# Chained attention, routed experts and dense layer: the TensorE expert loop and its exit rearranged, with one read and some subtractions moved

## The chip, the cores and the metric

The kernel runs on one core of one Trainium2 chip. The metric is the device time of one execution in microseconds (us). Before the change it is 740.41 us, the median of 3 runs (739.77 to 741.19).

## The reference, cut to what matters

Three layers follow each other. The first is a linear attention with decay (4 batches, 8 heads, 768 steps, head width 48), which gives 3072 rows of 384 numbers. The second is a routed layer of 8 experts, the third a dense layer:

```python
# second layer: x is (3072, 384); w1 (8, 384, 1024); w2 (8, 1024, 384)
do_compute = (x @ w_skip) > 0
e_idx = argmax(xc @ w_gate)                  # xc: the rows with do_compute
h = maximum(xc[mask] @ w1[e], 0)             # for each expert e
y[mask] = gate_w[mask] * (h @ w2[e])
out[do_compute] = xc + y
# third layer: w_in (384, 2048), w_out (2048, 384)
h = x @ w_in
g = h * clip(h + 3, 0, 6) / 6
result = g @ w_out
```

## The kernel before, in words

Every engine has a program of its own; they meet at semaphores only. All large products are made of three fp32r products of high and low parts: `three` (L866 to L869) issues high times high (L867), high times low (L868) and low times high (L869). A high part is made by ScalarE (a copy that rounds), a low part by VectorE (raw minus high).

**Stage 1** (about 0 to 170 us) is the attention and the routing. It writes the rows x to the scratch tensor `x_scratch` and counts how many tiles of 256 rows the experts need. With these inputs the plan has 8 tiles, one for each expert: the hidden products L867 into `bank_A` stand in the profile 144 times, which is 18 for each tile.

**Stage 2** (about 170 to 316 us) is the expert loop. Each engine runs `expert_loop` (L290): two tiles written out (j = 0 and 1), a loop over j = 2 to 7 by pairs, and behind a test `n_tiles > 8` a second loop for tiles 8 to 19, which is jumped over here. In the TensorE program one tile (`experts`, L880) has three parts: the hidden products for 8 pieces f, `rows_T` (L871), which transposes the gathered rows of the next tile, and the products with w2 for the two halves t = 0 (`bank_L`) and t = 1 (`bank_P`). That is 126 products in a tile. SyncE (`experts`, L368) reads the weights of tile j: w1 into `raw1` in three transfers (L378) once VectorE has made all low parts of w1 of tile j - 1, and w2 into `raw2` in one (L380) once the low parts of w2 of tile j - 1 are there. POOL gathers the rows of tile j + 1 (L505, two indirect transfers) and scatters the results of tile j (L537). VectorE evicts the results of a half with `yg` (L1222), ScalarE turns `raw1` into w1_hi (L659).

Behind the loop SyncE reads w_in into `wi_raw` (L388, eight transfers), waits for POOL's `s_before_last` (the scatters of the tile before the last have landed), reads the first 512 rows of x into `m_first` (L391, four transfers), and then reads w_out into `wo_raw` (L394, eight transfers of 384 KB).

**The passage to stage 3** is what the change is about. The rows of the last tile are not read back from `x_scratch`. TensorE transposes `m_first` (L961, 4 x 3 products, into the banks `bank_rT`, `bank_YT`, `bank_X`) and adds the last tile's results to them: `gain_hi` and `gain_lo` of the halves t = 0, 1, multiplied with the 0/1 matrix `goes_to` (L968, 12 products of 512 columns). Its order is t outside, then high and low, then the three banks kc, and each bank's `s_mT` is given at its last product. ScalarE makes `gain_hi` (L714) once both halves have been evicted (L1222), VectorE `gain_lo` (L1256). Then ScalarE makes `mT_hi` for each kc (L682) and VectorE `mT_lo` (L1230), and the first dense block may begin. ScalarE has before that made w_in's high parts 0 to 11 (`win_hi`, L646). VectorE makes w_in's low part 0 (`win_lo`, L1179) ahead of the three `mT_lo` and part 1 behind them.

**Stage 3** (about 331 to 745 us) is the dense layer in 6 blocks of 512 rows, each over 16 pieces f: 9 products of 512 columns for piece f of the hidden layer (it waits for `s_wilo` in the first block), then 12 products of 384 columns with w_out for piece f - 2 (`second`, L917). In the first block VectorE also makes w_out's low part f (L1184) and w_in's low part f + 2, and ScalarE w_out's high part f (L650) and w_in's high part f + 12. ScalarE waits for the whole of w_out (`s_wo`, L698) before the first of these.

Of the kernel before, what the change touches and what calls it, by code (L numbers as in the profile page):

```python
# [12 lines left out]
P = 128  # L13
B, H, S, HD = 4, 8, 768, 48
D = H * HD
# [5 lines left out]
KC = D // P  # L21
E, F1 = 8, 1024
G1 = F1 // P
F2 = 2048
G2 = F2 // P
TT = 256
TH = TT // P
MAXT = (N + E * (TT - 1)) // TT
# [6 lines left out]
BT = BLK // P  # L35
# [7 lines left out]
C_W1, C_W2 = (1, 2, 3), (1, 2, 3, 4)  # L43
W2_PARTS = len(C_W2)
W_PARTS = 8
HI_FIRST, LO_FIRST = 12, 2
SETS = 3
LATE = 3
GW = 32
# [14 lines left out]
def wait(eng, sem, value):  # L64

    if isinstance(value, int) and value <= 0:
        return
    eng.wait_ge(sem, value)


def chained_moe_program(nc, r, k, v, w, u, w_skip, w_gate, w1, w2, w_in, w_out, out, x_dram, slot_dram):
    ctx = ExitStack()
    with ctx:
# [90 lines left out]
        m_first = nc.alloc_sbuf_tensor_at("m_first", [P, BT, D], F32, offset=at_hi)  # L164
# [3 lines left out]
        goes_to, gain_hi, gain_lo = [], [], []  # L168
# [7 lines left out]
        wo_raw = nc.alloc_sbuf_tensor_at("wo_raw", [P, G2, D], F32, offset=at_lo)  # L176
# [6 lines left out]
        class Region:  # L183
# [60 lines left out]
        g = [de(f"g{i}", [P, BLK]) for i in range(2)]  # L244
# [45 lines left out]
        def expert_loop(eng, n_tiles, step):  # L290

            for i in range(2):
                step(i, 0, i)
            with eng.Fori(1, E // 2) as m:
                for i in range(2):
                    step(m * 2 + i, m, i)
            with eng.If(n_tiles > E):
                with eng.Fori(E // 2, MAXT // 2) as m:
                    for i in range(2):
                        step(m * 2 + i, m, i)  # L300
# [15 lines left out]
        def _(eng):  # L316
# [23 lines left out]
            for c in range(NC):  # L340
                for b in range(B):
                    n = c * B + b
# [22 lines left out]
            eng.dma_start(who_all[:, :, :], slots_by_p).then_inc(s_who_all, 16)  # L365
            n_tiles = tiles_planned(eng)

            def experts(j, m, i):  # L368
                if isinstance(j, int) and j == 0:
                    return  # L370
                with eng.If(n_tiles > j):
                    e = eng.value_load(plan[0:1, bass.ds(j, 1)], min_val=0, max_val=E - 1)
                    wait(eng, s_w1lo, KC * j)
                    if isinstance(j, int) and j == 1:
                        for done in s_xg[0]:
                            eng.wait_ge(done, 16)
                    for kc in range(KC):
                        eng.dma_start(raw1[:, kc, :], w1[bass.ds(e, 1), kc * P:(kc + 1) * P, :].rearrange("a p f -> p (a f)")).then_inc(s_raw1[kc], 16)  # L378
                    wait(eng, s_w2lo, G1 * j)
                    eng.dma_start(raw2[:, :, :], w2[bass.ds(e, 1), :, :].rearrange("a (g p) n -> p (a g) n", p=P)).then_inc(s_raw2, 16)  # L380

            expert_loop(eng, n_tiles, experts)

            wi_dram = w_in.rearrange("(k p) f -> p k f", p=P)
            wo_dram = w_out.rearrange("(g p) n -> p g n", p=P)
            for part in range(W_PARTS):
                own_f = slice(part * F2 // W_PARTS, (part + 1) * F2 // W_PARTS)
                eng.dma_start(wi_raw[:, :, own_f], wi_dram[:, :, own_f]).then_inc(s_wi, 16)  # L388
            eng.wait_ge(s_before_last, 1)
            for t in range(BT):  # L390
                eng.dma_start(m_first[:, t, :], x_dram[t * P:(t + 1) * P, :]).then_inc(s_m0[t], 16)  # L391
            for part in range(W_PARTS):
                own_g = slice(part * G2 // W_PARTS, (part + 1) * G2 // W_PARTS)
                eng.dma_start(wo_raw[:, own_g, :], wo_dram[:, own_g, :]).then_inc(s_wo, 16)  # L394
            eng.wait_ge(s_moe, 1)

            def load_m(blk):
# [323 lines left out]
        def _(eng):  # L721
# [144 lines left out]
            def three(dst, a_hi, a_lo, b_hi, b_lo, start, stop):  # L866
                eng.matmul(dst, a_hi, b_hi, start=start, stop=False)  # L867
                eng.matmul(dst, a_hi, b_lo, start=False, stop=False)  # L868
                return eng.matmul(dst, a_lo, b_hi, start=False, stop=stop)  # L869

            def rows_T(j, m, i):  # L871

                wait(eng, s_gTlo, TH * j)
                for t in range(TH):
                    eng.wait_ge(s_xg[i][t], 16 * (m + 1))
                    for kc in range(KC):
                        a = eng.transpose(p_xgT[t][:, kc * P:(kc + 1) * P], xg[i][:, t, kc * P:(kc + 1) * P], ident[:, :])
                    a.then_inc(s_gT, 1)

            def experts(j, m, i):  # L880
                with eng.If(n_tiles > j):
                    eng.wait_ge(s_w1lo, KC * (j + 1))
                    eng.wait_ge(s_gTlo, TH * (j + 1))
                    for f in range(G1):

                        wait(eng, s_hlo, G1 * j + (f - 1 if f < 2 else f - 2))
                        for kc in range(KC):
                            piece = slice(f * P, (f + 1) * P)
                            a = three(p_h[f % 3][:, 0:TT], w1_hi[:, kc, piece], w1_lo[:, kc, piece],
                                      xgT_hi[:, kc, :], xgT_lo[:, kc, :], kc == 0, kc == KC - 1)  # L890
                        a.then_inc(s_h, 1)
                    with eng.If(n_tiles > j + 1):
                        rows_T(j + 1, m + i, 1 - i)
                    for t in range(TH):
                        wait(eng, s_y2ev, TH * j + t + 1 - TH)
                        for f in range(G1):
                            if t == 0:
                                eng.wait_ge(s_hlo, G1 * j + f + 1)
                                eng.wait_ge(s_w2lo, G1 * j + f + 1)
                            tok = slice(t * P, (t + 1) * P)  # L900
                            a = three(p_y[t][:, 0:D], hT_hi[:, f, tok], hT_lo[:, f, tok], w2_hi[:, f, :], w2_lo[:, f, :],
                                      f == 0, f == G1 - 1)
                        if t < TH - 1:
                            a.then_inc(s_y2t, 1)
                    a.then_inc(s_y2, 1)

            rows_T(0, 0, 0)
            n_tiles = tiles_planned(eng)
            expert_loop(eng, n_tiles, experts)

            def rows_mT(kc, done):
                eng.wait_ge(s_mlo, done)
# [42 lines left out]


            eng.sem_inc(s_O, SHIFT)
            for t in range(BT):
                eng.wait_ge(s_m0[t], 16)
                for kc in range(KC):  # L960
                    eng.matmul(p_first_mT[kc][:, t * P:(t + 1) * P], m_first[:, t, kc * P:(kc + 1) * P], ident[:, :], start=t == 0, stop=False,  # L961
                               is_transpose=True, skip_group_check=True)
            for t in range(TH):
                for gain, done in ((gain_hi, s_gain_hi), (gain_lo, s_gain_lo)):
                    eng.wait_ge(done, t + 1)
                    final = gain is gain_lo and t == TH - 1
                    for kc in range(KC):
                        a = eng.matmul(p_first_mT[kc], gain[t][:, kc * P:(kc + 1) * P], goes_to[t][:, :], start=False, stop=final,  # L968
                                       skip_group_check=True)
                        if final:  # L970
                            a.then_inc(s_mT, 1)
            dense_loop(eng, blocks)


# [1 line left out]
        def _(eng):  # L976
# [198 lines left out]
            def win_lo(f):  # L1175

                piece = slice(f * P, (f + 1) * P)
                eng.wait_ge(s_wihi, f + 1)
                eng.tensor_tensor(wi_lo[:, :, piece], wi_raw[:, :, piece], wi_hi[:, :, piece].bitcast(F32), ALU.subtract).then_inc(s_wilo, 1)  # L1179
# [74 lines left out]
            for t in range(TH):  # L1254
                eng.wait_ge(s_gain_hi, t + 1)
                eng.scalar_tensor_tensor(gain_lo[t][:, :], p_y[t][:, 0:D], last_w[:, t:t + 1], gain_hi[t][:, :].bitcast(F32),  # L1256
                                         ALU.mult, ALU.subtract).then_inc(s_gain_lo, 1)
            win_lo(0)
            for kc in range(KC):
                rows_lo(0, kc, kc, p_first_mT[kc])  # L1260
            for f in range(1, LO_FIRST):
                win_lo(f)
            dense_loop(eng, blocks)

# [22 lines left out]
```

## Time and profile before

| | |
|---|---|
| median of 3 runs | 740.41 us |
| the profiled execution | 747.21 us |
| its span, first to last instruction | 745.4 us |
| TensorE busy with products | 699.1 us (94%) |
| VectorE / ScalarE / POOL busy | 385.0 / 323.6 / 140.5 us |
| mean granted clock of TensorE | 0.981 of full speed |
| moved by DMA | 65.61 MB, 88 GB/s on average |

The profiled execution is 1.8 us longer than its span and 6.8 us longer than the median of the runs without the profiler. PE is TensorE with its products, PEld its weight loads, DVE is VectorE, ACT ScalarE, SPq the queue of SyncE, POOLq that of POOL. Times in the trace are counted from the first instruction. "Idle before" is what an engine sat idle ahead of an instruction, with what ended it. "issue" stands where it waited for nothing that the profile shows.

### The profile page before, as it was taken

The numbers are of one execution on the slowest core, as the hardware profiler recorded it, in microseconds if no ns is written. First come the engines' busy times: TensorE is split into PE (matmuls) and PEld (weight loads), VectorE is DVE, ScalarE is ACT, GpSimd is POOL, SyncE is SP. The second block draws the span as 40 slices with busy tenths as digits, with TensorE's granted clock in tenths as the row PEclk, the third lists the DMA queues.
The fourth block names the chain that finished last, engine by engine and source line by source line (L and its number), as shares of the span: only waits on it lengthen the run. The fifth ranks groups of instructions, "written<-read, shape, count | busy, mean of one in ns | idle before, by whom it ended". The sixth has DMA issues, their size and how long they took to land.

```text
span 745.4 us, 13560 instructions
## 1 busy us (share of the span) xinstructions
PE 699.1 (94%) x5103; PEld 637.9 (86%) x5103; DVE 385.0 (52%) x767; ACT 323.6 (43%) x703; POOL 140.5 (19%) x189
## 2 busy tenths in 40 slices
PE   5999999938999999959999999999999999999997
PEld 3888888827999999948999899899998999998996
DVE  5576667565888888526554333333243333333332
ACT  3766666624555555625443233333232333323222
POOL 8647866441222222100000000000000000000000
PEclk9999999977999999989999999999999999999999
DMA  9888887113666666930002000200010020001001
GB/s 156 150 182 168 180 159 151 44 36 113 207 213 224 214 218 217 320 128 2 0 1 85 1 0 1 85 1 0 24 63 1 0 85 1 1 0 43 1 1 42
DMA packets 106988, 65.61 MB, mean 88 GB/s; under 512 B 79938, under 2 KB 102756, under 8 KB 106928
## 3 DMA queue, kind: packets, MB, share of 16 engines
q1 hardware_dynamic: 102864, 60.18, 30.4%
q0 software_dynamic: 2816, 4.60, 2.0%
q8 instruction: 39, 0.64, 0.4%
q10 hardware_dynamic: 1248, 0.02, 0.1%
q14 instruction: 21, 0.17, 0.1%
HBM read 53.69 MB, written 12.80 MB: 89 GB/s over the span
## 4 chain that ended last, share of the span: by engine, by line
PE 84%; ACT 4%; issue 4%; DVE 3%; DMA 2%; another core or an unknown queue 1%; POOL 1%; POOLq 0%; DVEq 0%; ACTq 0%; SPq 0%
PE bank_A L868 8%; PE bank_A L869 8%; PE bank_A L867 8%; PE bank_A L805 4%; PE bank_L L867 4%; PE bank_L L869 4%; PE bank_L L868 4%; PE bank_P L869 4%; PE bank_P L868 4%; PE bank_P L867 4%; PE bank_kT L868 3%; PE bank_kT L869 3%; PE bank_kT L867 3%; ACT bank_A L588 3%; PE bank_YT L869 3%
## 5 line engine op out<-in xcount | busy, mean ns | idle before, releaser
L1239 DVE TENSOR_TENSOR g_lo<-g,g_hi 128x512 fp32r<-128x512 f32 x96 | 66.5, 692 | 67.1 <-ACT g_hi L693 67.1
L693 ACT ACTIVATE g_hi<-g 128x512 fp32r<-128x512 f32 x96 | 60.7, 632 | 72.7 <-DVE g L1237 72.7
L1237 DVE SCALAR_TENSOR_TENSOR g<-cut,bank_A 128x512 f32<-128x512 f32 x60 | 41.2, 687 | 92.1 <-ACT cut L690 92.1
L690 ACT ACTIVATE cut<-bank_A 128x512 f32<-128x512 f32 x60 | 35.8, 597 | 102.3 <-PE bank_A L869 101.8
L867 PE MATMUL bank_A<-mT_hi,wi_hi 128*128 128x512 f32 x180 | 70.1, 389 | 1.8 <-DVE wi_lo L1179 1.8
L869 PE MATMUL bank_A<-mT_hi,wi_lo 128*128 128x512 f32 x180 | 71.0, 395 | 0.0
L868 PE MATMUL bank_A<-mT_lo,wi_hi 128*128 128x512 f32 x180 | 70.9, 394 | 0.0
L588 ACT ACTIVATE bank_A<-ident,own 128x128 f32<-128x128 f32 x192 | 59.2, 358 | 6.2 <-DVE A_sb L1030 3.2
L1237 DVE SCALAR_TENSOR_TENSOR g<-cut,bank_kT 128x512 f32<-128x512 f32 x36 | 24.8, 688 | 68.0 <-ACT cut L690 68.0
L690 ACT ACTIVATE cut<-bank_kT 128x512 f32<-128x512 f32 x36 | 21.5, 597 | 71.6 <-PE bank_kT L869 71.6
L1030 DVE TENSOR_TENSOR A_sb<-bank_A,upto 128x512 f32<-128x512 f32 x48 | 30.9, 685 | 23.7 <-PE bank_A L805 18.3
L867 PE MATMUL bank_kT<-mT_hi,wi_hi 128*128 128x512 f32 x108 | 42.1, 390 | 1.0 <-DVE mT_lo L1230 1.0
L867 PE MATMUL bank_A<-xgT_hi,w_hi 128*128 128x256 f32 x144 | 41.6, 289 | 1.3 <-DVE xgT_lo L1196 1.3
L869 PE MATMUL bank_kT<-mT_hi,wi_lo 128*128 128x512 f32 x108 | 42.7, 396 | 0.0
L868 PE MATMUL bank_kT<-mT_lo,wi_hi 128*128 128x512 f32 x108 | 42.6, 395 | 0.0
L672 ACT ACTIVATE hT_hi<-bank_A 128x256 fp32r<-128x256 f32 x48 | 18.4, 383 | 55.2 <-PE bank_A L869 54.2
L869 PE MATMUL bank_A<-xgT_hi,w_lo 128*128 128x256 f32 x144 | 41.5, 288 | 0.0
L868 PE MATMUL bank_A<-xgT_lo,w_hi 128*128 128x256 f32 x144 | 41.5, 288 | 0.0
L867 PEld LDWEIGHTS bank_A<-mT_hi,wi_hi 128*128 128x128 f32 x180 | 33.8, 188 | 7.9 <-issue 2.2
L869 PEld LDWEIGHTS bank_A<-mT_hi,wi_lo 128*128 128x128 f32 x180 | 33.7, 187 | 7.2
L868 PEld LDWEIGHTS bank_A<-mT_lo,wi_hi 128*128 128x128 f32 x180 | 33.8, 188 | 6.0
L805 PE MATMUL bank_A<-rT,kT 64*128 64x128 f32 x384 | 28.8, 290 | 8.3 <-ACT bank_A L588 5.7
(240 smaller groups left out, 1853.1 us busy)
## 6 DMA issues: line engine op xcount, KB each, us to landing
raw<-in_moe_w_dram SPq DMA_DIRECT2D x24, 512.0 KB
raw<-in_moe_w_dram SPq DMA_DIRECT2D x7, 1536.0 KB
r_in<-in_r_dram SPq DMA_DIRECT2D x24, 192.0 KB, 4.5
k_in<-in_k_dram SPq DMA_DIRECT2D x24, 192.0 KB, 4.5
v_in<-in_v_dram SPq DMA_DIRECT2D x24, 192.0 KB, 3.6
x_scratch<-y_sb SPq DMA_DIRECT2D x24, 192.0 KB, 2.5
out_dram<-o_sb SPq DMA_DIRECT2D x12, 384.0 KB, 2.8
m_in<-x_scratch SPq DMA_DIRECT2D x5, 768.0 KB, 5.4
```

The source lines that it names most:

```text
L588: a = eng.activation(p_A[:, o, q * P:(q + 1) * P], ident[:, :], ACT.Copy, scale=own[n % 2][:, 2 * q + o:2 * q + o + 1])
L672: eng.activation(hT_hi[:, f, :], p_h[f % 3][:, 0:TT], ACT.Relu).then_inc(s_hhi, 1)
L690: eng.activation(cut[f % 2][:, :], p_H[f % 3][:, :], ACT.Relu, bias=0.5, scale=1.0 / 6.0).then_inc(s_cut, 1)
L693: eng.activation(g_hi[f % 4][:, :], g[f % 2][:, :], ACT.Copy).then_inc(s_ghi, 1)
L805: m = eng.matmul(p_A[:, o, q * P:(q + 1) * P], kT[i][half, q, :], rT[i][half, q, :], start=False, stop=True, skip_group_check=True)
L867: eng.matmul(dst, a_hi, b_hi, start=start, stop=False)
L868: eng.matmul(dst, a_hi, b_lo, start=False, stop=False)
L869: return eng.matmul(dst, a_lo, b_hi, start=False, stop=stop)
L1030: eng.tensor_tensor(A_sb[i][:, o, :, :], p_A[:, o, :].rearrange("s (q t) -> s q t", q=NPAIR), mask, ALU.mult).then_inc(s_Aev, 1)
L1237: eng.scalar_tensor_tensor(g[f % 2][:, :], cut[f % 2][:, :], 1.0, p_H[f % 3][:, :], ALU.min, ALU.mult).then_inc(s_g, 1)
L1239: eng.tensor_tensor(g_lo[f % 4][:, :], g[f % 2][:, :], g_hi[f % 4][:, :].bitcast(F32), ALU.subtract).then_inc(s_glo, 1)
```

## The change: what it does

It does five things. (1) TensorE no longer uses `expert_loop`: tile 0 and tile 1 are written out, and one loop over pairs follows for m = 1 to 9, with the tests `n_tiles > 2m` and `n_tiles > 2m + 1` inside it, so with 8 tiles the passes m = 4 to 9 find nothing to do. The other engines keep `expert_loop`. (2) The transposes of `m_first` stand inside the tile, behind its last product, under the test `n_tiles < j + 2`. (3) The gain products run kc outside: all four of `bank_rT`, `s_mT`, then the next bank. (4) SyncE reads w_out behind the weights of tile 1 rather than behind `m_first`. (5) VectorE makes four low parts of w_in ahead of `mT_lo`, two behind, and in the first block the part f + 6.

```diff
-HI_FIRST, LO_FIRST = 12, 2
+HI_FIRST, LO_EARLY, LO_FIRST = 12, 4, 6
...
@@ SyncE, experts(j, m, i)
                     wait(eng, s_w2lo, G1 * j)
                     eng.dma_start(raw2[:, :, :], ...).then_inc(s_raw2, 16)
+                if isinstance(j, int):
+                    for part in range(W_PARTS):
+                        own_g = slice(part * G2 // W_PARTS, (part + 1) * G2 // W_PARTS)
+                        eng.dma_start(wo_raw[:, own_g, :], wo_dram[:, own_g, :]).then_inc(s_wo, 16)
...
             for t in range(BT):
                 eng.dma_start(m_first[:, t, :], x_dram[t * P:(t + 1) * P, :]).then_inc(s_m0[t], 16)
-            for part in range(W_PARTS):
-                own_g = slice(part * G2 // W_PARTS, (part + 1) * G2 // W_PARTS)
-                eng.dma_start(wo_raw[:, own_g, :], wo_dram[:, own_g, :]).then_inc(s_wo, 16)
...
@@ TensorE
+            def first_rows_T():
+                for t in range(BT):
+                    eng.wait_ge(s_m0[t], 16)
+                    for kc in range(KC):
+                        eng.matmul(p_first_mT[kc][:, t * P:(t + 1) * P], m_first[:, t, kc * P:(kc + 1) * P], ident[:, :], start=t == 0, stop=False,
+                                   is_transpose=True, skip_group_check=True)
...
             def experts(j, m, i):
-                with eng.If(n_tiles > j):
...
                     a.then_inc(s_y2, 1)
+                with eng.If(n_tiles < j + 2):
+                    first_rows_T()
...
-            expert_loop(eng, n_tiles, experts)
+            experts(0, 0, 0)
+            with eng.If(n_tiles > 1):
+                experts(1, 0, 1)
+            with eng.Fori(1, MAXT // 2) as m:
+                with eng.If(n_tiles > m * 2):
+                    experts(m * 2, m, 0)
+                    with eng.If(n_tiles > m * 2 + 1):
+                        experts(m * 2 + 1, m, 1)
...
             eng.sem_inc(s_O, SHIFT)
-            for t in range(BT):
-                eng.wait_ge(s_m0[t], 16)
-                ...
-            for t in range(TH):
-                for gain, done in ((gain_hi, s_gain_hi), (gain_lo, s_gain_lo)):
-                    eng.wait_ge(done, t + 1)
-                    final = gain is gain_lo and t == TH - 1
-                    for kc in range(KC):
-                        ...
+            for kc in range(KC):
+                for t in range(TH):
+                    for gain, done in ((gain_hi, s_gain_hi), (gain_lo, s_gain_lo)):
+                        eng.wait_ge(done, t + 1)
+                        a = eng.matmul(p_first_mT[kc], gain[t][:, kc * P:(kc + 1) * P], goes_to[t][:, :], start=False,
+                                       stop=gain is gain_lo and t == TH - 1, skip_group_check=True)
+                a.then_inc(s_mT, 1)
...
@@ VectorE
-            win_lo(0)
+            for f in range(LO_EARLY):
+                win_lo(f)
             for kc in range(KC):
                 rows_lo(0, kc, kc, p_first_mT[kc])
-            for f in range(1, LO_FIRST):
+            for f in range(LO_EARLY, LO_FIRST):
                 win_lo(f)
```

## Rows read from the trace of the kernel before

**Rows 1.** The page: span and busy time of each engine.

```profile
span 745.4 us, 13560 instructions
PE 699.1 (94%) x5103; PEld 637.9 (86%) x5103; DVE 385.0 (52%) x767; ACT 323.6 (43%) x703; POOL 140.5 (19%) x189
```

**Rows 2.** Windows: length, busy time of each engine, clock, DMA share, GB/s.

```profile
400.00:745.00 345.00, 340.52 (x1735) 308.65 (x1734) 123.37 (x184) 109.45 (x184) 0.00 (x0) 1.00 0.07 23
316.40:330.80 14.40, 6.18 (x26) 4.96 (x25) 3.07 (x6) 2.53 (x5) 0.97 (x1) 0.76 0.52 177
190.00:194.00 4.00, 4.00 (x27) 4.00 (x27) 2.52 (x7) 0.00 (x0) 1.04 (x1) 1.00 1.03 350
```

**Rows 3.** Waits of TensorE: waited for, us in total, times, longest.

```profile
PE bank_X L961 <- issue: 3.7, 1, 3.7
PE bank_rT L961 <- issue: 3.5, 1, 3.5
PE bank_A L867 <- DVE wi_lo L1179: 1.8, 1, 1.8
PE bank_kT L877 <- DMA xg<-x_scratch,who: 1.2, 1, 1.2
```

**Rows 4.** Timeline of TensorE at the passage: start, duration, instruction, idle before.

```profile
316.07 0.34 PE L869 MATMUL bank_P<-w_hi,hT_lo 128*128 128x384 f32 x1
319.86 0.30 PE L961 MATMUL bank_rT<-ident,m_first 128*128 128x128 f32 x1 [3.45 <-issue]
...
324.32 0.37 PE L961 MATMUL bank_X<-ident,m_first 128*128 128x128 f32 x1 [3.72 <-issue]
...
329.36 0.39 PE L968 MATMUL bank_X<-goes_to,gain_lo 128*128 128x512 f32 x1
...
332.71 0.40 PE L869 MATMUL bank_kT<-mT_hi,wi_lo 128*128 128x512 f32 x1
```

**Rows 5.** Timelines of VectorE and ScalarE at the passage.

```profile
316.45 0.62 DVE L1222 SCALAR_TENSOR_TENSOR yg<-bank_P,who,xg 128x384 f32<-128x384 f32 x1 [3.47 <-PE bank_P L869]
318.25 0.61 DVE L1256 SCALAR_TENSOR_TENSOR gain_lo<-bank_P,last_w,gain_hi 128x384 fp32r<-128x384 f32 x1
318.77 0.55 DVE L1179 TENSOR_TENSOR wi_lo<-wi_raw,wi_hi 128x384 fp32r<-128x384 f32 x1
329.95 0.69 DVE L1230 TENSOR_TENSOR mT_lo<-bank_rT,mT_hi 128x512 fp32r<-128x512 f32 x1 [10.63 <-ACT mT_hi L682]
...
329.32 0.60 ACT L682 ACTIVATE mT_hi<-bank_rT 128x512 fp32r<-128x512 f32 x1 [11.17 <-PE bank_rT L968]
```

**Rows 6.** DMA queue q8 (packets, MB, share): span, then 175 to 246, 317 to 326 us.

```profile
q8 instruction: 39, 0.64, 0.4%
...
q8 instruction: 4, 0.07, 0.4%
...
q8 instruction: 2, 0.03, 1.5%
```

**Rows 7.** Timelines of SyncE's queue and of ScalarE around tiles 1 and 2.

```profile
185.55 0.39 SPq L380 DMA_DIRECT2D raw<-in_moe_w_dram  x1
189.58 1.37 SPq L378 DMA_DIRECT2D raw<-in_moe_w_dram  x3
...
202.46 2.94 ACT L659 ACTIVATE w_hi<-raw 128x1024 fp32r<-128x1024 f32 x3
```

**Rows 8.** POOL's second gather for tile 2, its reader, DMA landings 193:211, 175:246, 299:317.

```profile
198.10 1.00 POOL L505 DMA_INDIRECT xg<-x_scratch,who  x1 [0.31 <-issue]
...
201.89 0.49 PE L877 MATMUL bank_kT<-ident,xg 128*128 128x128 f32 x3
...
xg<-x_scratch,who POOLq DMA_INDIRECT x2, 2.9
...
x_scratch<-yg,whom POOLq DMA_INDIRECT x7, 4.0
...
x_scratch<-yg,whom POOLq DMA_INDIRECT x3, 6.3
```

More of the change, by code:

```diff
@@ L366, in _ @@
             n_tiles = tiles_planned(eng)
+            wo_dram = w_out.rearrange("(g p) n -> p g n", p=P)
             def experts(j, m, i):
@@ L380, in experts @@
                     eng.dma_start(raw2[:, :, :], w2[bass.ds(e, 1), :, :].rearrange("a (g p) n -> p (a g) n", p=P)).then_inc(s_raw2, 16)
+                if isinstance(j, int):
+                    for part in range(W_PARTS):
+                        own_g = slice(part * G2 // W_PARTS, (part + 1) * G2 // W_PARTS)
+                        eng.dma_start(wo_raw[:, own_g, :], wo_dram[:, own_g, :]).then_inc(s_wo, 16)
             expert_loop(eng, n_tiles, experts)
             wi_dram = w_in.rearrange("(k p) f -> p k f", p=P)
-            wo_dram = w_out.rearrange("(g p) n -> p g n", p=P)
             for part in range(W_PARTS):
@@ L878, in rows_T @@
                     a.then_inc(s_gT, 1)
-            def experts(j, m, i):
-                with eng.If(n_tiles > j):
-                    eng.wait_ge(s_w1lo, KC * (j + 1))
-                    eng.wait_ge(s_gTlo, TH * (j + 1))
-                    for f in range(G1):
-                        wait(eng, s_hlo, G1 * j + (f - 1 if f < 2 else f - 2))
-                        for kc in range(KC):
[L888 to L893, printed above, removed]
-                    for t in range(TH):
[L895 to L905, printed above, removed]
@@ new lines, in first_rows_T @@
+            def first_rows_T():
[4 more added lines that the diff above has]
+                                   is_transpose=True, skip_group_check=True)
+            def experts(j, m, i):
+                eng.wait_ge(s_w1lo, KC * (j + 1))
+                eng.wait_ge(s_gTlo, TH * (j + 1))
+                for f in range(G1):
+                    wait(eng, s_hlo, G1 * j + (f - 1 if f < 2 else f - 2))
+                    for kc in range(KC):
+                        piece = slice(f * P, (f + 1) * P)
+                        a = three(p_h[f % 3][:, 0:TT], w1_hi[:, kc, piece], w1_lo[:, kc, piece],
+                                  xgT_hi[:, kc, :], xgT_lo[:, kc, :], kc == 0, kc == KC - 1)
+                    a.then_inc(s_h, 1)
+                with eng.If(n_tiles > j + 1):
+                    rows_T(j + 1, m + i, 1 - i)
+                for t in range(TH):
+                    wait(eng, s_y2ev, TH * j + t + 1 - TH)
+                    for f in range(G1):
+                        if t == 0:
+                            eng.wait_ge(s_hlo, G1 * j + f + 1)
+                            eng.wait_ge(s_w2lo, G1 * j + f + 1)
+                        tok = slice(t * P, (t + 1) * P)
+                        a = three(p_y[t][:, 0:D], hT_hi[:, f, tok], hT_lo[:, f, tok], w2_hi[:, f, :], w2_lo[:, f, :],
+                                  f == 0, f == G1 - 1)
+                    if t < TH - 1:
+                        a.then_inc(s_y2t, 1)
+                a.then_inc(s_y2, 1)
+                with eng.If(n_tiles < j + 2):
+                    first_rows_T()
@@ L957, in _ @@
             eng.sem_inc(s_O, SHIFT)
-            for t in range(BT):
-                eng.wait_ge(s_m0[t], 16)
[L960 to L963, printed above, removed]
-                for gain, done in ((gain_hi, s_gain_hi), (gain_lo, s_gain_lo)):
-                    eng.wait_ge(done, t + 1)
-                    final = gain is gain_lo and t == TH - 1
[L967 to L971, printed above, removed]
+            for kc in range(KC):
+                for t in range(TH):
+                    for gain, done in ((gain_hi, s_gain_hi), (gain_lo, s_gain_lo)):
[3 more added lines that the diff above has]
+                a.then_inc(s_mT, 1)
             dense_loop(eng, blocks)
```

## The prediction

> **What bounds the kernel now.** I read the page first: TensorE is busy with products for 94% of the span, no other engine for more than 52% [rows 1]. So a microsecond is won only where TensorE stands still or runs slowly. The windows show where that is: from 400 us on it misses 4.5 of 345 us at full clock, and in tiles 0 to 7 hardly anything, but between 316.4 and 330.8 us it is busy for 6.2 of 14.4 us, at a mean clock of 0.76 [rows 2]. That is the passage from the last expert tile to the dense layer. The waits say what it stood for there: twice, 3.5 and 3.7 us, for nothing that the profile shows ("issue"), both at the transposes of `m_first`; later 1.8 us for w_in's low part of piece 2 [rows 3].
>
> An engine that waits for nothing may be waiting for its own code. The queue q8 carries 39 packets and 0.64 MB [rows 6], 16 KB each. Products and weight loads together are 2 x 5103 instructions [rows 1], so q8 carries 63 bytes for each: it is TensorE's code, brought in blocks. Four packets came in 175 to 246 us, one for each tile; none in 246 to 317 us, when the loop ran its second and third pass; and two in 317 to 326 us [rows 6], just where the two stalls are. A pass of two tiles is then held while it repeats, and the jump over the unused second loop, about 36 KB of code by the count of its products, lands outside what is held. The first block arrives at 319.86, five transposes run, and the next one is missing until 324.32 [rows 4].
>
> **The change, part by part.** I call the end of the last tile E: its last product starts at 316.07 and ends at 316.41 [rows 4].
>
> (1) and (2), the loop and the transposes. The transposes follow the last product in the same piece of code, so they run at once: five took from 319.86 to 320.60 (324.32 less the stall of 3.72), 0.3 us for one and 0.11 for each further one [rows 4]; 12 end at about 317.9. Then the sequencer makes six empty passes. No row shows the price of one. From below it is nothing seen: TensorE crosses a tile's tests and branches without a gap, since its queue is full. From above I take the 3.7 us of a missing block [rows 3] for each. I take it near the lower end, below 0.5 us, because the blocks of the loop's head and tail are both held when the loop ends, as they were in passes two and three [rows 6]. The cover: the last half tile is 24 products, 4.2 us, which need only been issued, and the gains aren't ready before 317.7. The sequencer should be through the tile's code at about 313, so 4.6 us are there for six passes, or 0.75 us each, at no cost. If that cover is gone, every further 0.1 us a pass costs 0.6 us. The Trainium skill prices a branch (Advanced Engine Details and Errata, Control Flow Timing) at about 51 ns, with a comparison at 108 ns; six passes of two each would by that estimate be 1.9 us, which no run here shows.
>
> The chain to the dense layer, then, is that of the gains. `yg` of the second half runs at 316.45, the last `gain_lo` at 318.25 to 318.86 [rows 5]; the change touches neither. **(3)** With kc outside, three of bank 0's four gain products are done by then, and the last ends at about 319.35 (0.39 us, as at 329.36 [rows 4]). ScalarE's `mT_hi` takes 0.60: 320.0. **(5)** VectorE now makes four low parts first, from 318.77, of 0.47 us each in a row (0.55 alone [rows 5]): 320.65, so `mT_lo` 0 is done at 321.35 rather than 320.65, and 1 and 2 at 0.61 us intervals, 322.0 and 322.6. The other eight gain products end at 321.2, also before the first `mT_lo`: the new order costs nothing, VectorE sets the pace. The nine products of piece 0 start at 321.5 and the last three after `mT_lo` 2: piece 0 ends at 323.6. Before, its last product started at 332.71 and ended at 333.1 [rows 4]. **Saved: 9.5 us.** In it are the two stalls (7.2 us [rows 3]), and the half clock that followed them: with TensorE idle for some 1 us in place of 7, I expect the clock to stay at 2.4 GHz.
>
> In the first block, piece 2 waited 1.8 us for its low part, which stood behind those of block 0's `g` on VectorE [rows 3]. Parts 0 to 5 now exist before, and f + 6 is made in the same slots, so the wait goes. Next in line is w_out's low part 0, needed after piece 2; VectorE reaches it some 1 us before TensorE does. **Saved: 1.8 us.**
>
> (4) w_out. Where it was, it filled the DMA queues during the passage; that is part of why the blocks came late. Where it goes, eight transfers of 384 KB, 3.1 MB, stand in SyncE's program behind the issue at 185.55 and ahead of the wait and the three w1 transfers of tile 2, now issued at 189.58 [rows 7]. At the 350 GB/s of that stretch [rows 2] w_out takes 9 us. The queue then holds w2 of tile 1 (1.6 MB), w_out and w1 of tile 2 (1.6 MB), 18 us with the gathers between them, so tile 2's w1 lands from 203 to 206.3; ScalarE wants it at 202.46 [rows 7]. High part 1.0, low part 1.2 and the gathered rows' low parts 1.0 behind it end at 209.5. TensorE wants them at 210.5, with 1 us to spare. The gather of tile 2 has nothing to spare: issued at 198.10, with 2.9 us to landing it is there at 201.0, and TensorE reads it at 201.89 [rows 8]. In a full queue a scatter lands after 6.3 us instead of 4.0 [rows 8]. The same 2.3 us here make 203.3, 1.4 us late, and TensorE stands for it with the second half of its tile behind. Bounds: nothing (the queue drains in time) and about 5 us (scatter, gather and w1 all late, as in tile 3 to 4, where a late gather cost 1.2 [rows 3]). I take **1.5 us lost**. The 0.6 us of issue time for each of the eight is SyncE's and hides nothing else.
>
> The sum: -9.5 - 1.8 + 1.5 = **-9.8 us**. Against the profiled execution, 747.2, that makes 737.4; its excess of 6.8 us over the median I leave alone, so the median goes from 740.4 to **730.6 us**.
>
> **The rivals.**
> *A. One code stall is left, or w_out costs its upper bound.* The exit of the loop may still need a block that isn't held, or VectorE's code may be late. That costs up to 3.7 us, less what the wait for the gains covers; with 5 us for w_out both give 730.6 + 3.7 + 3.5 = 737.8 at most, and 734 to 735 for either alone. For it: blocks came only one ahead of use (the second stall). Against: the code behind the loop follows it directly. Chance 0.20.
>
> *B. The empty passes fetch code: slower.* The pair is now about 39 KB, as each tile has 12 transposes more. It covers four blocks, and the one behind is fetched too. If only four are held, which is all that the trace proves, then each pass throws out what the next needs. Price: six passes at 3.7 us [rows 3] are 22.3 us, from 313 to 335.4. Then 12 gain products at the half clock and piece 0 end at about 342.7, against 333.1 before: +9.6 - 1.8 + 1.5, about 749.7 us. It decides at 0.75 us a pass, and turns the sum positive at about 2.3 us a pass. Against it: no packet in three passes, the last with a fourth block already brought. The Trainium skill (Runtime: NRT & Kernel Launch, Instruction fetch mechanics) has a rule that speaks for it: a taken branch whose target lies outside a window of two blocks forces a fetch. By this rule each empty pass would fetch at both its jumps, twice the price, 772 us; but the trace disagrees, with a 36 KB loop repeated without a packet. Chance of both forms 0.05.
>
> *C. The stalls are not the code's place but its volume.* If the passage needs two blocks at 3.6 us wherever it stands, only the 1.8 us and the lighter queue are won, and w_out's price is paid: about 739.5 to 741. For it: the second stall came when the DMA was emptying. Against: the transposes now lie in blocks that have run. Chance 0.04.
>
> **How the numbers follow.** The forecast as summed has 0.71, with 728 to 733 as its own range: w_out at nothing, and a clock that saves 1 us more, below; 2 us more for w_out or the passes above. Rival A reaches 737.8. I take 728.0 to 738.0, which leaves out B, C and a tail. A measurement of this kernel tells 0.2%, 1.5 us, from no change. Faster by more: 0.92; within: 0.03 (most of C); slower: 0.05 (B).
>
> **What would show it.** Right: the "issue" waits at the transposes gone, these directly behind the last product of `bank_P`; clock near 1 in the 14 us behind E; first product with `mT_hi` some 5 us behind E (before 14.4); no wait on `wi_lo`; DMA full from 187 to about 205 us, with a wait on `xg` in tile 1 of 1 to 2 us. Wrong: q8 packets inside the expert loop after its first pass, or several at its end (B); an "issue" wait ahead of the gain products (A); TensorE waiting at the start of tile 2 for `w_lo` or `xgT_lo` (w_out dearer than I think).

## The result, and the profile after

The changed kernel takes 737.39 us (median of 5 runs, 736.86 to 737.46) against 741.14 us before (5 runs, 739.77 to 741.64): a ratio of 0.9952, 95% interval [0.9938, 0.9967]. That is 3.7 us faster, where 9.8 us had been forecast. The sign and the range held; the size of the gain did not.

The two profiled executions differ by 9.8 us all the same, 745.4 against 735.6 us of span. That is a trap. The first product of tile 0 (before, then after) shows it:

```profile
173.18 0.55 PE L867 MATMUL bank_A<-xgT_hi,w_hi 128*128 128x256 f32 x1 [1.26 <-DVE xgT_lo L1196]
```

```profile
166.62 0.55 PE L869 MATMUL bank_A<-xgT_hi,w_hi 128*128 128x256 f32 x1 [1.26 <-DVE xgT_lo L1207]
```

6.6 of the 9.8 us lie in stage 1, whose code the change does not touch. Of these, 4.5 us are waits of TensorE for ScalarE's `diagonal` (L588 before, L590 after), first before, then after:

```profile
PE bank_A L805 <- ACT bank_A L588: 5.7, 10, 1.1
```

```profile
PE bank_A L807 <- ACT bank_A L590: 1.2, 3, 0.5
```

Tile 0 starts at 166.6 us in this one trace and at 172.5 to 176.0 in the other thirteen of both kernels and their variants. What sets it was not found. The three later comparisons ran on three chips, and before takes 747 to 748 us in all of them; on which chip the first comparison ran is not recorded. So each experiment is read against the before of its own comparison, and by stretches of the trace.

I cut each trace at three points: the first product of tile 0, the end E of tile 7's last product, and the first product with w_out. What follows that product takes 406.3 to 406.4 us in every trace, before included. The stretches, from the timeline of TensorE (us):

| | tile 0 to E | first gain product | end of piece 0 | first w_out product |
|---|---|---|---|---|
| before, first profile | 143.2 | E + 9.2 | E + 16.7 | E + 22.7 |
| before, second profile | 142.9 | E + 8.5 | E + 16.2 | E + 22.2 |
| changed | 148.1 | E + 3.65 | E + 10.6 | E + 14.5 |
| changed, second profile | 148.2 | E + 3.65 | E + 10.6 | E + 14.5 |

So the expert stage lost 4.9 us, and the passage up to the first w_out product won 8.2. The sum is 3.3 us, near the 3.7 of the medians.

Not all of the 4.9 us is the change's doing. In every trace tile 0 begins at a granted clock of 0.5, which lasts 4.0 to 6.1 us from its first product: 4.7 in the first profile of before, 5.5 in that of the changed kernel. TensorE works at half pace for that long, so for this reason alone the stage can differ by about 1 us between two traces. It takes 142.9 to 143.9 us in the eight traces where w_out is read elsewhere, and 147.4 to 148.2 in the six where it is read behind tile 1. The means are 4.4 us apart. The first 10 us of tile 0, before and then after (columns as in [rows 2]; the granted clock is the third number from the end):

```profile
173.18:183.18 10.00, 10.00 (x66) 10.00 (x67) 5.65 (x12) 4.91 (x13) 0.00 (x0) 0.77 0.39 150
166.62:176.62 10.00, 10.00 (x63) 10.00 (x64) 5.30 (x12) 4.79 (x12) 0.00 (x0) 0.73 0.41 154
```

**The passage after**, TensorE's timeline (the rows that answer to [rows 4]):

```profile
314.41 0.34 PE L871 MATMUL bank_P<-w_hi,hT_lo 128*128 128x384 f32 x1
314.59 0.27 PE L887 MATMUL bank_rT<-ident,m_first 128*128 128x128 f32 x1
...
315.79 0.27 PE L887 MATMUL bank_X<-ident,m_first 128*128 128x128 f32 x1
318.40 0.47 PE L980 MATMUL bank_rT<-goes_to,gain_hi 128*128 128x512 f32 x1 [2.34 <-issue]
...
319.41 0.63 PE L980 MATMUL bank_rT<-goes_to,gain_lo 128*128 128x512 f32 x1
...
324.95 0.39 PE L871 MATMUL bank_kT<-mT_hi,wi_lo 128*128 128x512 f32 x1
...
329.27 0.33 PE L869 MATMUL bank_YT<-wo_hi,g_hi 128*128 128x384 f32 x1
```

The first transpose starts 0.18 us behind the start of the last product, and both stalls of [rows 3] are gone. A new one of 2.34 us stands ahead of the gain products. It is of the kind "issue" again, although the gains were ready: the last `gain_lo` ends at 317.20. Most of the gain products then start 0.43 us apart, not 0.23: the granted clock is 0.5 from 318.85 to 322.3 us. VectorE (the rows that answer to [rows 5]) no longer sets the pace:

```profile
316.59 0.61 DVE L1267 SCALAR_TENSOR_TENSOR gain_lo<-bank_P,last_w,gain_hi 128x384 fp32r<-128x384 f32 x1
317.12 1.95 DVE L1190 TENSOR_TENSOR wi_lo<-wi_raw,wi_hi 128x384 fp32r<-128x384 f32 x4
320.71 0.69 DVE L1241 TENSOR_TENSOR mT_lo<-bank_rT,mT_hi 128x512 fp32r<-128x512 f32 x1 [1.64 <-ACT mT_hi L684]
```

**The expert stage after.** The gather of tile 2 comes late. TensorE's timeline, the landings of 179 to 205 us, and two windows (columns as in [rows 2]) show it:

```profile
197.79 0.52 PE L879 MATMUL bank_rT<-ident,xg 128*128 128x128 f32 x3 [2.29 <-DMA xg<-x_scratch,who]
```

```profile
xg<-x_scratch,who POOLq DMA_INDIRECT x2, 6.8
```

```profile
197.00:199.00 2.00, 0.89 (x7) 0.69 (x7) 0.00 (x0) 0.15 (x1) 0.00 (x0) 1.00 1.04 398
199.00:203.00 4.00, 4.00 (x16) 4.00 (x15) 3.06 (x3) 3.74 (x5) 0.00 (x0) 0.57 1.03 371
```

The gather takes 6.8 us to landing instead of 2.9 [rows 8]. TensorE stands for 2.3 us, and for another 0.3 at the second half. Behind this the granted clock is 0.57 on the mean of 4 us, in a part of the tile where it had been 1: 3.4 us at half clock, in which 1.7 us are lost. Together that is 4.3 of the 4.4 us. The transposes of successive tiles start 20.06 and 19.74 us apart here, 17.6 in a tile that nothing disturbs.

Code: q8 has 37 packets in the changed kernel for 39 before.

### The profile page after: what moved, and what is told of

It is laid out like the page before. It is cut to its first block, busy times and chain, and to the rows that moved or that the text cites. A ratio compares the mean times of both kernels' runs of the same rounds, so it can differ in the third digit from the quotient of the medians.

```text
span 735.6 us, 13594 instructions
## 1 busy us (share of the span) xinstructions
PE 700.2 (95%) x5103; PEld 639.5 (87%) x5103; DVE 383.7 (52%) x767; ACT 324.3 (44%) x703; POOL 141.0 (19%) x189
## 4 chain that ended last, share of the span: by engine, by line
PE 90%; DVE 2%; DMA 2%; ACT 2%; issue 2%; POOL 1%; POOLq 0%; DVEq 0%; SPq 0%; ACTq 0%
PE bank_A L870 8%; PE bank_A L871 8%; PE bank_A L869 8%; PE bank_A L807 4%; PE bank_L L869 4%; PE bank_L L871 4%; PE bank_L L870 4%; PE bank_P L871 4%; PE bank_P L870 4%; PE bank_P L869 4%; PE bank_kT L870 3%; PE bank_kT L871 3%; PE bank_kT L869 3%; PE bank_YT L871 3%; PE bank_YT L870 3%; PE bank_YT L869 3%
## 5 line engine op out<-in xcount | busy, mean ns | idle before, releaser
L590 ACT ACTIVATE bank_A<-ident,own 128x128 f32<-128x128 f32 x192 | 59.1, 359 | 5.5 <-DVE A_sb L1041 3.0
L1218 DVE TENSOR_TENSOR w_lo<-raw,w_hi 128x384 fp32r<-128x384 f32 x64 | 35.9, 561 | 0.0
```

Of the source, the lines that this page charges most:

```text
L590: a = eng.activation(p_A[:, o, q * P:(q + 1) * P], ident[:, :], ACT.Copy, scale=own[n % 2][:, 2 * q + o:2 * q + o + 1])
L1218: eng.tensor_tensor(w2_lo[:, f, :], raw2[:, f, :], w2_hi[:, f, :].bitcast(F32), ALU.subtract).then_inc(s_w2lo, 1)
```

## The experiments

**1. The kernel before, again** (no edit).

> The kernel before, unchanged, for a second profile. Theory T: its profiled execution of before was 6.6 us long in stage 1 by chance (first hidden product of tile 0 at 173.18 us against 166.62 us in the changed kernel, the waits of L805 for ScalarE 5.7 us against 1.2), and the change itself is worth 3 to 4 us. Then the time is the same as before within 0.2%, the span about 739, tile 0 starts at about 166.6, and both issue stalls at the transposes are there, 7 us together. Rival R: the issue stalls were long by chance in that one execution. Then tile 0 starts near 173 here too and the stalls come to less than 4 us.

Measured: 747.71 us against 747.14 (1.0007 [0.9995, 1.0018]); tile 0 starts at 174.82, the issue stalls are 3.55 and 2.90 us. The stalls are no accident of one execution, as T had it. But stage 1 is as long here as in the first profile, in this kernel and in the others of the comparison (173.3 to 173.9): that part of T missed. It is the profile of the changed kernel that has the short stage 1. The timed runs of before in the first comparison (739.8 to 741.6 us) lie 6 us under its profiled execution of 747.2, so they probably have it short too; no trace shows it, and why was not tried.

**2. w_out back at its old place**, in the changed kernel.

```diff
@@ SyncE, experts(j, m, i)
-                if isinstance(j, int):
-                    for part in range(W_PARTS):
-                        own_g = slice(part * G2 // W_PARTS, (part + 1) * G2 // W_PARTS)
-                        eng.dma_start(wo_raw[:, own_g, :], wo_dram[:, own_g, :]).then_inc(s_wo, 16)
@@ SyncE, behind the reads of m_first
+            for part in range(W_PARTS):
+                own_g = slice(part * G2 // W_PARTS, (part + 1) * G2 // W_PARTS)
+                eng.dma_start(wo_raw[:, own_g, :], wo_dram[:, own_g, :]).then_inc(s_wo, 16)
```

> The changed kernel with part 4 undone: w_out is read behind m_first again. Theory T: w_out behind tile 1 costs 4.9 us of the expert stage (from tile 0's first product to the end of tile 7 143.2 us before, 148.1 after), and the passage no longer needs a quiet DMA since its code is held. Then this takes about 732.5 us, 8 to 9 below before, with no wait of the transposes and no wait on xg in tile 1 over 0.5 us. Rival R: it was the w_out traffic at the passage that made the passage slow, so with it there again the issue wait before the gain products grows from 2.3 to 4 us or more and the time is 736 us or more.

Measured: 738.74 us against 747.14, 0.9887 [0.9871, 0.9904], 8.4 us below before. Tile 0 to E is 143.7 us, and the stall ahead of the gain products is 2.34 us to the hundredth. With the code in place, w_out's traffic costs the passage nothing: piece 0 ends at E + 9.0 here and also where w_out is out of the way (experiment 4). The time is over R's 736 us, but only because before is longer here too (see 4); R's longer stall did not come.

**3. w_out behind tile 1 alone**, in the kernel before.

```diff
@@ SyncE, experts(j, m, i), behind the read of raw2
+                if isinstance(j, int):
+                    for part in range(W_PARTS):
+                        own_g = slice(part * G2 // W_PARTS, (part + 1) * G2 // W_PARTS)
+                        eng.dma_start(wo_raw[:, own_g, :], wo_dram[:, own_g, :]).then_inc(s_wo, 16)
@@ SyncE, behind the reads of m_first
-            for part in range(W_PARTS):
-                own_g = slice(part * G2 // W_PARTS, (part + 1) * G2 // W_PARTS)
-                eng.dma_start(wo_raw[:, own_g, :], wo_dram[:, own_g, :]).then_inc(s_wo, 16)
```

> The kernel before with part 4 alone: w_out behind tile 1, all else as before. Theory T: the expert stage is 4.9 us longer as in the changed kernel; the two issue stalls stay, each shorter by at most 1 us since the fetches meet no w_out traffic. Then 743.5 to 746 us, 2.5 to 5 slower than before. Rival R: the two stalls come from the w_out traffic, so they shrink to under 2 us together and the time is 740 to 741 us, no difference.

Measured: 747.31 us, 1.0004 [0.9992, 1.0015]: no difference, the time of R, by another sum than either gave. Tile 0 to E is 147.4 us, 4.5 more; but piece 0 ends at E + 12.3, 3.9 less than in the second profile of before. The stalls, from TensorE's timeline:

```profile
321.56 0.30 PE L963 MATMUL bank_rT<-ident,m_first 128*128 128x128 f32 x1 [0.67 <-issue]
...
324.52 0.34 PE L963 MATMUL bank_X<-ident,m_first 128*128 128x128 f32 x1 [2.22 <-issue]
```

The first stall had been 3.45 and 3.55 us in the two profiles of before. q8's packet for it starts at E - 1.9 here, and at E + 0.8 and E + 0.9 there; from its start to the first transpose it is 2.6 to 2.7 us in all three. So w_out's read in the full queues did not make the rest of the fetch longer, it made the packet start 2.7 to 2.8 us later. q8 in this trace from 318 to 320 us (E is at 320.89; before had its first packet behind E [rows 6]):

```profile
q8 instruction: 1, 0.02, 3.2%
```

The second stall (2.22 us, before 3.72 and 2.90) doesn't fall as clearly: it is 2.17 us in experiment 11, where w_out's read is back at the passage, and in the first profile the DMA share is 0.02 in the middle of it (322 to 324 us). T had given the lighter traffic at most 2 us.

**4. w_out at the end of stage 1**, in the changed kernel.

```diff
@@ SyncE, stage 1, the loop over c and b, behind store and load_v; the read behind tile 1 goes
+                    if c == NC - 1:
+                        for part in (2 * b, 2 * b + 1):
+                            own_g = slice(part * G2 // W_PARTS, (part + 1) * G2 // W_PARTS)
+                            eng.dma_start(wo_raw[:, own_g, :], wo_dram[:, own_g, :]).then_inc(s_wo, 16)
```

> The changed kernel with w_out read at the end of stage 1, two parts behind each batch of the last chunk, where the DMA share is 0.01 to 0.2. Theory T: nothing waits for the DMA there, and the expert stage is back at 143.2 us: about 732.5 us, the same as with w_out at its old place or up to 0.5 us less. Rival R: the reads delay the last stores of x or the slot scatters, so that tile 0 starts 2 us or more later than 166.6 us; the time is then 734.5 us or more.

Measured: 738.85 us against 747.14, 0.9898 [0.988, 0.9915], as in 2. Tile 0 to E is 143.2 us, the gathers of tile 2 land after 3.1 us, and tile 0 starts at 173.34, no later than in the others. The absolute 732.5 of experiments 2 and 4 was reckoned from the 737.4 of the first comparison and not carried over to this chip's before; as a difference to before it is 8.6, and 8.3 to 8.4 came by the medians (7.6 here by the ratio). By its absolute numbers R would have come true, but only because stage 1 is 7 us longer on this chip in every variant. T stands.

**5. The changed kernel, again** (no edit).

> The changed kernel itself, beside the others of this batch. Before takes about 747.1 us on this chip. Theory T: the change is worth the same 3.5 us as in the first comparison, stage 1 is 6 to 7 us longer here for both. Then 743 to 744 us, the wait of 2.3 us ahead of the gain products and a wait on xg of 2 to 3 us in tile 1. Rival R: the gain of 3.5 us depends on the execution, because the clock fell during the gain products in that one trace (0.43 us for a product of 512 columns instead of 0.23, 2 us in all). Then 741.5 us or less here, with the gain products at 0.23 us.

Measured: 742.85 us against 747.93, 0.9933 [0.9917, 0.9949], 5.1 us below before, between the two theories. Its passage is that of the first profile to 0.02 us, half clock and all:

```profile
327.87 0.47 PE L980 MATMUL bank_rT<-goes_to,gain_hi 128*128 128x512 f32 x1 [2.34 <-issue]
```

Against experiment 2 the change is 3.3 us short by what each gained here, 4.8 by the ratio of the first comparison. The traces give 6.0 us: 4.4 in the expert stage and 1.6 at the passage. Why the medians give less is not shown.

**6. No empty passes**, in the changed kernel.

```diff
-            with eng.Fori(1, MAXT // 2) as m:
-                with eng.If(n_tiles > m * 2):
+            with eng.If(n_tiles > 2):
+                with eng.Fori(1, (n_tiles + 1) // 2) as m:
```

> The changed kernel with the loop over pairs ended at (n_tiles + 1) // 2, so that there are no empty passes. Theory T: the wait of 2.3 us ahead of the gain products is TensorE's sequencer in six empty passes of about 1 us each. Then the wait goes, the first gain product runs within 0.3 us of the last transpose or of gain_hi, piece 0 of the first block ends 1.4 us sooner, and the time is 1.4 to 3.5 us below the changed kernel (the upper end where its clock fell). Rival R: the wait is a code block that isn't held behind the loop. Then it stays at 2 us or more and the time is the same within 0.3 us.

Measured: 740.68 us against 747.93, 0.9906 [0.989, 0.9922], 2.2 us below the changed kernel (in the traces the passage is 3.2 us shorter, of which 1.6 are the clock, which stays at 1 here). The stall is gone; the gain products run as the gains come:

```profile
323.39 0.51 PE L980 MATMUL bank_rT<-goes_to,gain_lo 128*128 128x512 f32 x1 [0.15 <-DVE gain_lo L1267]
326.48 0.47 PE L869 MATMUL bank_kT<-mT_hi,wi_hi 128*128 128x512 f32 x1 [0.23 <-DVE mT_lo L1241]
```

Here VectorE does set the pace, as predicted, and piece 0 ends at E + 7.4, where the prediction had E + 7.2. The whole passage as summed was right, but for the passes.

**7. Twelve empty passes**, in the changed kernel.

```diff
-            with eng.Fori(1, MAXT // 2) as m:
+            with eng.Fori(1, MAXT // 2 + 6) as m:
```

> The changed kernel with six more empty passes (the loop over pairs ends at 16 instead of 10). Theory T: each costs about 1 us, so the wait ahead of the gain products grows from 2.3 to about 8.3 us and the time by 6 us. Rival R1: the passes are hidden or below 0.5 us each, and the wait is something else; then the time grows by less than 3 us. Rival R2: each fetches a block, at 3 us; then it grows by 18 us.

Measured: 748.62 us against 747.93, 5.8 us above the changed kernel. In the trace:

```profile
330.07 0.76 PE L980 MATMUL bank_rT<-goes_to,gain_hi 128*128 128x512 f32 x1 [6.75 <-issue]
```

The first gain product moves from E + 3.65 to E + 8.06, 4.41 us for six passes: 0.735 us each. q8 has 37 packets as before this edit, so no pass fetches code. Counted back from E + 3.65, the first six passes begin at E - 0.8, if a pass costs the same there. That is assumed: the granted clock is 0.5 from 326.3 us on, so most of the six added passes fall in a stretch at half clock, while the first six had a clock of 1. The other 1.5 us of the medians aren't in the passage; tile 0's start differs by more than that between executions.

**8. Gain products t outside**, in the changed kernel (part 3 undone).

```diff
-            for kc in range(KC):
-                for t in range(TH):
-                    for gain, done in ((gain_hi, s_gain_hi), (gain_lo, s_gain_lo)):
...
+            for t in range(TH):
+                for gain, done in ((gain_hi, s_gain_hi), (gain_lo, s_gain_lo)):
+                    eng.wait_ge(done, t + 1)
+                    final = gain is gain_lo and t == TH - 1
+                    for kc in range(KC):
...
```

> The changed kernel with part 3 undone: the gain products run t outside again. Theory T: as the gain products all stand behind the empty passes with their inputs ready, the new order gives bank 0 after 4 products instead of 10 and so lets ScalarE and VectorE start 6 products sooner, 1.4 us at 0.23 us each. Undone, mT_hi 0 starts that much later, and the time is 1 to 2 us above the changed kernel. Rival R: VectorE's four low parts or the end of the 12 products set the pace either way; then the same within 0.3 us, as the prediction had it.

Measured: 744.91 us against 747.93, 0.9962 [0.9945, 0.9978], 2.1 us above the changed kernel in the median. The runs are wide apart here (741.97 to 747.93), so the trace decides. Its clock stays at 1 at the passage, where that of the changed kernel fell, so it is compared with experiments 2 and 4, which have the same clock and kc outside. Piece 0 ends at E + 10.0 here and at E + 9.0 there. The order is worth 1.0 us where the gains are ready before the products, as they are behind the empty passes. The prediction had given it nothing.

**9. w_out in stage 1 and no empty passes** (the edits of 4 and 6 together).

> The changed kernel with w_out read in stage 1 and no empty passes. Theory T: the two prices are independent, 4.9 us of the expert stage and 1.6 us at the passage (full clock) add up. Tile 0 to end of tile 7 takes 143.2 us, piece 0 of the first block ends 7.2 to 7.5 us behind E, and the time is about 10 us below before on the same chip (before 747: 737). Rival R: something else bounds the passage once the passes are gone (the gains, VectorE's low parts), and w_out in stage 1 alone was already worth all of it; then 8.3 us below before, as with w_out moved alone.

Measured: 736.17 us against 748.06, 0.9849 [0.9829, 0.987]. Tile 0 to E 143.5 us, piece 0 ends at E + 7.4, first w_out product at E + 11.3. By the ratio that is 11.3 us below before; the trace gives 10.9 for the passage (22.2 less 11.3). T holds, with 1 us more than it gave, and this version is faster than both kernels.

**10. As 9, gain products t outside, two low parts ahead of mT_lo.**

```diff
-HI_FIRST, LO_EARLY, LO_FIRST = 12, 4, 6
+HI_FIRST, LO_EARLY, LO_FIRST = 12, 2, 6
```

The gain products are as in experiment 8.

> As e9_both, with the gain products t outside again and two instead of four low parts of w_in ahead of mT_lo (four behind). Theory T: without empty passes the gain products run as the gains come, so t outside lets them end about 1.4 us sooner (E + 3.4 instead of 4.8), and mT_lo 0 is ready at E + 4.3 instead of 5.0. The first dense product then starts 0.6 to 0.8 us sooner than in e9_both and the time is 0.5 to 0.8 us lower. Rival R: no difference within 0.3 us, as ScalarE's or VectorE's chain sets the pace in both.

Measured: 736.90 us against 748.06, 0.9848 [0.983, 0.9866], the same as 9. A miss for T: the 12 products take 3.0 us here, so they end at E + 4.35, not 3.4. Bank 0 gets its last product only in the last group of three, and ScalarE and VectorE come behind it: `mT_lo` 0 is ready at E + 5.3, not 4.3, and piece 0 ends at E + 7.7.

**11. The low parts alone**, in the kernel before (part 5).

```diff
-HI_FIRST, LO_FIRST = 12, 2
+HI_FIRST, LO_EARLY, LO_FIRST = 12, 4, 6
...
-            win_lo(0)
+            for f in range(LO_EARLY):
+                win_lo(f)
             for kc in range(KC):
                 rows_lo(0, kc, kc, p_first_mT[kc])
-            for f in range(1, LO_FIRST):
+            for f in range(LO_EARLY, LO_FIRST):
```

> The kernel before with part 5 alone (four low parts of w_in ahead of mT_lo, two behind, f + 6 in the block). Theory T: the four are hidden by the code stalls and the wait of piece 2 goes, from the end of piece 0 to the first product with w_out 3.9 instead of 6.0 us: 2.0 us below before (about 0.27%). Rival R: the wait only moves to another piece or to w_out's low part; then the same as before within 0.5 us.

Measured: 746.04 us against 748.06, 0.9977 [0.9965, 0.9988], 1.7 to 2.0 us. End of piece 0 to the first w_out product is 3.9 us, as in the changed kernel. T holds.

**12. w_out in stage 1 alone**, in the kernel before (the edit of 4).

> The kernel before with w_out read in stage 1 and nothing else changed. Theory T: the two code stalls at the passage stay, but as fetches without w_out traffic: the end of piece 0 comes about 12.3 us behind E (as with w_out behind tile 1) instead of 16.2 to 16.7, with the expert stage at 143.2 us. Then 4 us below before (0.5%). Rival R: the stalls shortened with w_out behind tile 1 only because the expert stage ended later against an unrelated event; then less than 1 us below before.

Measured: 742.97 us against 748.06, 0.9931 [0.9915, 0.9948], 5.2 us. Tile 0 to E 143.7, piece 0 ends at E + 10.9. TensorE's timeline:

```profile
317.21 0.30 PE L962 MATMUL bank_rT<-ident,m_first 128*128 128x128 f32 x1 [0.52 <-issue]
...
320.57 0.27 PE L962 MATMUL bank_X<-ident,m_first 128*128 128x128 f32 x1 [2.62 <-issue]
```

The first stall, 3.5 us before, is 0.5 here: q8's packet for it starts at 314.7 us (E - 2.0), so TensorE still has products to run while it comes. The second stays. T holds, with 1 us more than it gave: the granted clock stays at 1 here, while it fell to 0.5 in before and in experiment 3, and the gain products take 3.0 us, not 4.0 as in 3.

## Why the prediction was right or wrong

**The sum** was -9.8 us, the result -3.7. Two terms and one cover failed, and all lie on the side of less gain: w_out 3.4 us, the passage 3.4 us, less 0.2 that the low parts gave on top. By the traces that leaves 3.2 of the 9.8.

*w_out: "I take 1.5 us lost".* The expert stage got 4.9 us longer, 4.4 on the mean of all traces. The mechanism was the one named, the gather of tile 2 in a full queue, but the price was taken from a scatter (6.3 less 4.0 us [rows 8]), and the gather took 3.9 us longer, not 2.3. The stall was 2.6 us instead of 1.4. And the stall was not all: the clock fell behind it, to 0.5 for 3.4 us, which cost another 1.7. I had reckoned with the clock at the passage and not here. The upper bound of "about 5 us" was right. Its support was not: the wait of 1.2 us on xg in [rows 3] belongs to the second half of tile 0's own gather, before the expert loop has filled, and not to tiles 3 to 4 as the text says. Of w1 of tile 2 the forecast was right: ScalarE waited 2.5 us for it (2.52 ahead of L661 at 198.85), and TensorE never stood for its low parts.

*The empty passes: "below 0.5 us each", "4.6 us are there for six passes", "at no cost".* A pass costs 0.735 us, near the 0.75 that would by my reckoning just have been free; but the cover was about 2.1 us, not 4.6, from E - 0.8 to the end of the transposes at E + 1.3, where the first gain product runs without the passes (experiment 6). I had taken TensorE's queue to be long enough for all 24 products of the half tile and the 12 transposes behind them, and no row had shown how far its sequencer runs ahead. The wait of 2.34 us is what came of it. The Trainium skill's prices (Advanced Engine Details and Errata, Control Flow Timing) gave an estimate of 1.9 us for all six; 4.4 us was measured for six more. What else a pass spends its time on was not taken apart.

*The passage: "Saved: 9.5 us".* It was 6.1 (16.7 less 10.6). Of the missing 3.4 us, 1.6 are the passes at full clock (E + 9.0 in experiments 2 and 4, E + 7.4 without passes), and 1.6 the half clock of most gain products: behind its idle 2.3 us the granted clock fell to 0.5 in both profiles of the changed kernel, and not in experiments 2, 4 and 8 with the same 2.34 us. "I expect the clock to stay at 2.4 GHz" was a step without a margin.

*"Saved: 1.8 us"* for the low parts: 2.0 us, right in place and size.

*"The new order costs nothing"*: right, and it even wins 1.0 us, since VectorE was not what set the pace.

**The stalls as code fetches** were read rightly: the transposes inside the held code have none, and q8 carries two packets less. That the transposes waited for `m_first` itself is ruled out: its last read was issued before 308.8 us and took at most 4.7 us to land, before E. "That is part of why the blocks came late", of w_out's traffic, was said and left out of the sum: experiment 12 shows that reading w_out at the end of stage 1 is by itself worth 5.2 us, by a first block that comes sooner and a clock that does not fall. So the gains of parts 1, 2 and 4 overlap. Either taking w_out out of the passage or keeping the transposes' code at hand wins most of it; the change pays for both, and the price of one was 4.4 to 4.9 us.

**The rivals.** A is what happened, with a cause that it did not name: a stall of the "issue" kind is left, and w_out costs its upper bound. It had 0.20 and gave 737.8 for both together. That this lies near the measured 737.4 is partly luck: no block was missing, and passes and half clock together happened to cost 3.2 us where A had 3.7 for a block. B fell: twelve passes fetch nothing. By the window of two blocks (the Trainium skill, Runtime: NRT & Kernel Launch, Instruction fetch mechanics) they would have; the trace disagrees with it also here, 4.4 us for six more passes and the same 37 packets. C fell too, although w_out's part in it was true.

## What to carry to other kernels

Two fixes of one stall don't add up: before paying for the second, try each alone, and look where in the whole run the DMA stands idle before moving a read into a loop that is already fed just in time (here stage 1's end was free, worth 5 us). An empty pass of this loop cost 0.7 us, and is free only under a lead that a row of the trace shows; end the loop at the count that is known at run time. Compare two profiles stretch by stretch before believing the difference of their spans: 6.6 us of the 9.8 here were of a stage that nobody had touched.

## What the runs showed of the hardware

An empty pass of a loop with one test cost TensorE's sequencer 0.735 us (experiment 7, most of it at a granted clock of 0.5), and its lead over the array was too short to hide six of them.

An idle TensorE was followed by a granted clock of 0.5 in some traces and not in others. In tile 1 it was idle for 2.1 to 2.3 us and again for 0.2 to 0.5, and the clock fell in all six traces. Ahead of the gain products it was idle for 2.34 us, and the clock fell in two of five traces (the changed kernel's two), at a cost of 1.6 us; it fell also in the one with twelve passes, idle for 6.75. What decides between them stays open. The place of w_out's read alone does not: it is behind tile 1 in experiment 8 too, and the clock stays at 1 there.

At the passage of the kernel before, TensorE waited for the first code block for 3.5 to 4.2 us where w_out was read there, and for 0.5 to 0.7 where it was read elsewhere (experiments 12 and 3). The transpose that needs the second block came 4.5, 3.6 and 3.1 us after the first transpose where w_out was read there (the two profiles of before, experiment 11), and 3.4 and 3.0 where it was not.

Indirect gathers of 128 rows, two to a tile, landed after 2.9 us at a DMA share of 0.2 to 0.5 (197 to 201 us in before) and after 6.8 us at a share of 1.
